# Fetching the row tags by a gather, and waits by block at the edge between two stages

## The chip, the cores and the metric

The kernel runs on one core of one Trainium2 chip. The metric is the device time of one execution in microseconds; the median of three runs stands for a kernel. The profiled execution is one more run, recorded by the hardware profiler. TensorE, VectorE, ScalarE, GpSimd and the queue engine SyncE (SP) each work through their own list of instructions and wait for each other by semaphores.

## The reference

```python
out = attention_scan(q, k, v, a_re, a_im)      # a complex decay scan over 768 steps, 16 heads of 48
x = out.reshape(1536, 384)
# switch layer: 8 experts, each token to its best one, at most 384 tokens per expert
logits = x @ w_gate;  expert = argmax(logits)
gate = softmax(logits)[expert]
h = relu(disp @ w1[e]);  y = h @ w2[e]          # disp: the rows kept by expert e, in order
x = gate * y[expert, pos] if kept else 0        # (1536, 384)
# bilinear layer
return ((x @ w_a) * (x @ w_b)) @ w_out          # 384 -> 1536 -> 384
```

All of it is float32. In the kernel each float32 operand of the large products is split into a high part (h) and the rest (l), and a product is three matmuls (h·h, l·h, h·l).

## The kernel before

Stage 1, up to about 236 us, computes the scan in chunks and the routing of every row. A row goes by an indirect DMA into a DRAM table `sorted_x[expert, rank]` of rows with 386 values: the 384 of x and two **tags**, the sum of the exponentials (its reciprocal is the gate value) and the row's number. Slots that no row takes hold 0 and a number out of range. `total` holds, per expert, how many rows it kept, and `fst`, the place of its first kept row when all kept rows are packed behind each other; `first` and `nkept` are integer copies.

Stage 2 works through the 8 experts. `hidden(e)` is the first product: 8 groups f of 9 matmuls (L1006) with 224 moving columns (384 where an expert has more rows), into four banks in turn; ScalarE writes hh = relu, VectorE hl, and between them they split w2. `outputs(e)` is the second product (L1041): for each f, three column blocks c of three matmuls, into banks 4, 5 and 6, and only after the last of the 72 does `act.wait(m_p)` let ScalarE copy yh and VectorE compute yl, block by block (L1066, L1068), into the packed arrays yh and yl at the column `first[e]`. After f = 1, 3 and 5 TensorE turns one tile of 128 rows of the next expert (`turn_tile`): L943 turns the two tag columns, L945 the three blocks of x. `split_tile` then copies xh (L951), the tags into `tags` at the next expert's place (L952), and xl (L955). Experts 0 to 5 are outputs of a hardware loop (`trip`), 6 follows it with the same body; each prepares the next expert.

SP's queue carries, in the order of the code: the rows of the next expert but one (L907), its w1 (L901) and its w2 (L904), each as soon as the buffer is free. Before the loop it carries w2 of expert 1 and `load_group(0)`, the first of six groups of weights of the bilinear layer.

The last expert's `outputs` turns no tiles. Behind its product TensorE turns `tags` back by 12 small transposes (L1151), and VectorE makes from them `back`, the row numbers, and `gate2`, the squared gate values (L1154 to L1157). All of TensorE's bilinear stage waits for the last yl (`pe.wait(m_y)`), ScalarE's for gate2.

Stage 3, the bilinear layer, takes the packed rows in three tiles of 512. For each of 12 groups f: 18 matmuls (L1208) for a and b, ScalarE copies a (L1221), VectorE multiplies by b (L1223), ScalarE and VectorE split the result (gh L1227, gl L1229), and `outs(f - 1)` adds to the output by 12 matmuls (L1181). In the first tile the weights are split alongside, in the order that they are needed. At the end of a tile ScalarE scales four blocks of 128 rows by gate2 (L1245), and GpSimd scatters each to its rows in DRAM by `back` (L1248).

Key lines around the edge between stages 2 and 3:

```python
            act.wait(m_p)                       # one mark: the whole second product
            for c in range(KC):
                m = act.done(ss.activation(yh[:, c, ...], bank[YB0 + c][:, 0:CAP], ACT.Copy))
...
        m_y = outputs(E - 1, True)
        pe.wait(m_tagged)
        for i in range(NT):
            m = nc.tensor.transpose(tag[:, i, :], tags[:, i * P:(i + 1) * P], ident[0:2, 0:2])
...
            act.wait(m_rows)
            pe.wait(m_y)
```

Of the kernel before, what the change touches and what calls it, by code (L numbers as in the profile page):

```python
# [68 lines left out]
def build(nc, dims, qk, v, a, w_gate, w1, w2, wa, wb, wo, out, CAP):  # L69
# [33 lines left out]
    with ctx:  # L103
# [9 lines left out]
        sorted_x = nc.dram_tensor("sorted_x", (E, N, ROW), F32, kind="Internal").ap()  # L113
        x_rows = nc.dram_tensor("x_rows", (P, L, C2), F32, kind="Internal").ap()
# [51 lines left out]
        with att:  # L166
# [706 lines left out]
            tags = sb("tags", [2, N + CAP], F32, at=exp_r, side="right")  # L873
            used = 2 * KC * (F + CAP) + XT_N * ROW
            assert 2 * KC * F2 <= used and used + N + CAP <= 3 * KC * F2 - GF * KC * P
            sb("apart", [P, 4 * KC * F2 - used - N - CAP], F32, at=exp_r, side="right")
# [51 lines left out]
        extra = sb("raw2", [P, 2 * GA + GO], F32, at=ctx)  # L928
        pool.wait(pe_done, dve_done)
# [33 lines left out]
        act.wait(m_tags)  # L963
# [4 lines left out]
        for i in range(XT_N):  # L968
            m_x0 = split_tile(i, bank[4 + i], m_t0[i], 0)
# [53 lines left out]
        def outputs(e, last):  # L1023
# [8 lines left out]
            m_p = (pe, pe.n + tiles + 1, pe.reg is not None)  # L1032
            m_t = [(pe, pe.n + i + 1, pe.reg is not None) for i in range(tiles)]
            m_x = [(dve, dve.n + 3 * i + 3, dve.reg is not None) for i in range(tiles)]

            def mm(cols):
                for f in range(NF):
                    pe.wait(m_h[f])
                    for c in range(KC):
                        for i, (wx, xx) in enumerate(((w2h, hh), (w2h, hl), (w2l, hh))):  # L1040
                            m = nc.tensor.matmul(bank[YB0 + c][:, 0:cols], wx[:, f, c * P:(c + 1) * P], xx[:, f, 0:cols],  # L1041
                                                 start=f == 0 and i == 0, stop=f == NF - 1 and i == 2)
# [8 lines left out]
            sized(n, mm)  # L1051
# [3 lines left out]
            else:  # L1055
                at_next = nc.scalar.value_load(first[0:1, bass.ds(e + 1, 1)], min_val=0, max_val=N)
                nc.scalar.wait_ge(s_w1, (e + 2) * 16)
                w1_marks[0] = []
                for f in range(NF):
                    w1_marks[0].append(split(*piece1(f)))  # L1060
                    if f % 2 and f // 2 < tiles:
                        assert split_tile(f // 2, bank[7], m_t[f // 2], at_next) == m_x[f // 2]
                row_marks[0] = (m_t[-1], m_x[-1])
            act.wait(m_p)
            for c in range(KC):
                m = act.done(ss.activation(yh[:, c, bass.ds(at_act, CAP)], bank[YB0 + c][:, 0:CAP], ACT.Copy))  # L1066
                dve.wait(m)
                m_y = dve.done(tt(yl[:, c, bass.ds(at_dve, CAP)], bank[YB0 + c][:, 0:CAP],  # L1068
                                  z32(yh[:, c, bass.ds(at_dve, CAP)]), ALU.subtract))
# [29 lines left out]
        load_group(0)  # L1099
        act.wait(m_y0)  # L1100
# [17 lines left out]
        nc_loop(nc, trip, E - 2, (pe, dve, act), {id(pe): NF + 1 + XT_N, id(dve): per, id(act): per + XT_N}, ENG)  # L1118
# [27 lines left out]
        m_tagged = (act, act.n, False)  # L1146
# [158 lines left out]
```

## Time and profile before

| | |
|---|---|
| median of 3 runs | 625.35 us (624.22 to 625.88) |
| profiled execution | 623.43 us, span 622.2 us |
| TensorE busy with matmuls | 560.4 us, 90% of the span |
| VectorE, ScalarE busy | 368.7 us (59%), 274.7 us (44%) |
| GpSimd busy | 40.5 us (7%) |
| mean granted TensorE clock | 0.969 |
| DMA traffic | 70.10 MB, 113 GB/s over the span |

The span runs from the first to the last instruction; the profiled time is the device time of the same execution. Matmuls are pipelined, so the busy time of TensorE is not time at its peak: what a group of them costs is read from start to start.

### The profile page before, as it was taken

The page shows a single profiled execution, that of the slowest core. Times are in us where ns is not written, and L with a number is a line of the kernel's source. Part 1 is how long each engine was busy: PE and PEld are TensorE (multiplying, and loading weights), DVE is VectorE, ACT ScalarE, POOL GpSimd, SP SyncE. Part 2 cuts the span into 40 slices and gives each one's busy share as a digit, 9 for nine tenths or more (in the row PEclk, how much of TensorE's full clock was granted, in tenths as well). Part 3 has the DMA queues.
Part 4 walks back from the last instruction along what each step waited for, and adds up shares of the span by engine and source line. Part 5 has one row for each costly group of instructions (what it writes and reads, how often), then busy time and mean ns, then how long its engine had stood idle before and what let it go on. Part 6 is the DMA issues. An engine that isn't in the chain of part 4 may idle for free.

```text
span 622.2 us, 10348 instructions
## 1 busy us (share of the span) xinstructions
PE 560.4 (90%) x3876; PEld 496.6 (80%) x3877; DVE 368.7 (59%) x910; ACT 274.7 (44%) x571; POOL 40.5 (7%) x51
## 2 busy tenths in 40 slices
PE   0564878899999986999999999999999999999996
PEld 0232555899999984999999998888888888888886
DVE  5999999777667645888888876444422222121211
ACT  5656475712222224777877775443332121321112
POOL 1000000001111116000000000000001000110002
PEclk9867899999999988999999999899999999999999
DMA  8990035493222115566677734222001000010001
GB/s 334 397 337 1 2 152 146 133 309 83 65 62 58 41 30 171 167 241 194 217 239 240 222 123 154 76 77 76 1 1 51 1 0 1 14 39 1 0 1 51
DMA packets 42201, 70.10 MB, mean 113 GB/s; under 512 B 12976, under 2 KB 35248, under 8 KB 41456
## 3 DMA queue, kind: packets, MB, share of 16 engines
q1 hardware_dynamic: 40624, 64.80, 31.7%
q0 software_dynamic: 1536, 4.73, 2.4%
q8 instruction: 28, 0.46, 0.3%
q14 instruction: 13, 0.11, 0.1%
HBM read 52.97 MB, written 16.55 MB: 112 GB/s over the span
## 4 chain that ended last, share of the span: by engine, by line
PE 80%; DVE 13%; ACT 3%; DMA 2%; issue 1%; POOL 0%; SPq 0%; DVEq 0%; ACTq 0%; POOLq 0%
PE psum L1208 25%; PE psum L1181 12%; PE psum L1006 10%; PE psum L1041 10%; PE psum L815 4%; PE psum L649 4%; PE psum L789 3%; DVE region L357 3%; PE psum L819 2%; PE psum L442 2%; DVE region L362 2%; PE psum L834 2%; PE psum L690 1%; DVE region L406 1%; PE psum L945 1%
## 5 line engine op out<-in xcount | busy, mean ns | idle before, releaser
L1223 DVE TENSOR_TENSOR ga<-ga,psum 128x512 f32<-128x512 f32 x36 | 24.8, 688 | 134.1 <-PE psum L1208 134.1
L1227 ACT ACTIVATE gh<-ga 128x512 fp32r<-128x512 f32 x36 | 22.8, 632 | 82.4 <-DVE ga L1223 77.9
L265 PE MATMUL psum<-region,ident 128*128 128x384 f32 (+1 forms) x42 | 23.3, 646 | 39.4 <-ACT region L275 28.4
L1221 ACT ACTIVATE ga<-psum 128x512 f32<-128x512 f32 x36 | 21.5, 598 | 76.3 <-PE psum L1208 76.3
L1041 PE MATMUL psum<-hh,w2h 128*128 128x224 f32 x192 | 54.1, 282 | 0.0
L1006 PE MATMUL psum<-xh,w1h 128*128 128x224 f32 x192 | 52.9, 275 | 1.3 <-DVE xl L955 1.3
L1006 PE MATMUL psum<-xh,w1l 128*128 128x224 f32 x192 | 52.8, 275 | 0.8 <-issue 0.8
L1006 PE MATMUL psum<-xl,w1h 128*128 128x224 f32 x192 | 52.7, 274 | 0.0
L1041 PE MATMUL psum<-hh,w2l 128*128 128x224 f32 x192 | 52.6, 274 | 0.0
L1041 PE MATMUL psum<-hl,w2h 128*128 128x224 f32 x192 | 52.5, 273 | 0.0
L265 PEld LDWEIGHTS psum<-region,ident 128*128 128x128 f32 x42 | 10.3, 262 | 48.6 <-issue 21.0
L1181 PE MATMUL psum<-woh,gh 128*128 128x384 f32 x144 | 48.6, 338 | 0.4 <-DVE gl L1229 0.2
L1181 PE MATMUL psum<-wol,gh 128*128 128x384 f32 x144 | 48.6, 337 | 0.0
L1181 PE MATMUL psum<-woh,gl 128*128 128x384 f32 x144 | 48.3, 336 | 0.0
L1208 PE MATMUL psum<-yh,wah 128*128 128x512 f32 x108 | 43.2, 400 | 1.5 <-DVE yl L1068 1.5
L1208 PE MATMUL psum<-yh,wal 128*128 128x512 f32 x108 | 43.2, 400 | 0.0
L1208 PE MATMUL psum<-yl,wah 128*128 128x512 f32 x108 | 43.1, 399 | 0.0
L1208 PE MATMUL psum<-yh,wbh 128*128 128x512 f32 x108 | 42.9, 398 | 0.0
L1208 PE MATMUL psum<-yl,wbh 128*128 128x512 f32 x108 | 42.8, 397 | 0.0
L1208 PE MATMUL psum<-yh,wbl 128*128 128x512 f32 x108 | 42.7, 395 | 0.0
L1229 DVE TENSOR_TENSOR gl<-ga,gh 128x512 fp32r<-128x512 f32 x36 | 25.0, 693 | 25.2 <-ACT gh L1227 25.2
L1006 PEld LDWEIGHTS psum<-xh,w1h 128*128 128x128 f32 x192 | 36.9, 192 | 1.6 <-DVE xl L955 1.6
(185 smaller groups left out, 1475.3 us busy)
## 6 DMA issues: line engine op xcount, KB each, us to landing
raw<-w SPq DMA_DIRECT2D x14, 1536.0 KB, 6.9
sorted_x<-region SPq DMA_DIRECT2D x8, 579.0 KB, 11.2
queries<-qk SPq DMA_DIRECT2D x4, 1152.0 KB, 17.4
xrow<-sorted_x SPq DMA_DIRECT2D x7, 579.0 KB, 3.9
region<-x_rows SPq DMA_DIRECT2D x14, 288.0 KB
queries<-w SPq DMA_DIRECT2D x2, 1536.0 KB, 10.8
x_rows<-region SPq DMA_DIRECT2D x5, 576.0 KB, 2.8
region<-a SPq DMA_DIRECT2D x2, 1152.0 KB, 8.6
```

What stands on the lines that cost most here:

```text
L265: nc.tensor.matmul(x, ident[:], x0[:, cut], start=True, stop=False)
L357: m.append(dve.done(tt(by[k_], walk(AT_Z[2] + prev + k_ * D, [-SA, 2], [0, 2], [1, D]), walk(AT_Z[0] + now + k_ * D, [SA, 2], [SA, 2], [1, ...
L649: m = nc.tensor.matmul(bank[2 + r][0:L, i * L:(i + 1) * L], XT[:, p, :], QT[:, p, :], start=True, stop=True)
L815: m = nc.tensor.matmul(bank[4 + r][0:L, i * D:(i + 2) * D], SC[r][:, i, :], twice(p), start=True, stop=j == 0)
L1006: m = nc.tensor.matmul(bank[b][:, 0:cols], wx[:, c, f * P:(f + 1) * P], xx[:, c, 0:cols], start=c == 0 and i == 0, stop=c == KC - 1 and i ...
L1041: m = nc.tensor.matmul(bank[YB0 + c][:, 0:cols], wx[:, f, c * P:(c + 1) * P], xx[:, f, 0:cols], start=f == 0 and i == 0, stop=f == NF - 1 ...
L1181: m = nc.tensor.matmul(ot[s][:, 0:DM], gx[f % GB3][:, s * P:(s + 1) * P], wx[:, f, :], start=f == 0 and i == 0, stop=f == NF2 - 1 and i == 2)
L1208: m = nc.tensor.matmul(b_[:, 0:TT], wx[:, f, c, :], xx[:, c, t * TT:(t + 1) * TT], start=c == 0 and i == 0, stop=c == KC - 1 and i == 2)
L1221: m = act.done(ss.activation(ga[f % 2][:], ba[:, 0:TT], ACT.Copy))
L1223: m = dve.done(tt(ga[f % 2][:], ga[f % 2][:], bb[:, 0:TT], ALU.mult))
L1227: m = act.done(ss.activation(gh[f % GB3][:], ga[f % 2][:], ACT.Copy))
L1229: m_g.append(dve.done(tt(gl[f % GB3][:], ga[f % 2][:], z32(gh[f % GB3][:]), ALU.subtract)))
```

## The change

The tags are no longer carried through TensorE. After expert 0's first product SP's queue copies them out of `sorted_x` into a small DRAM table `kept_tags` of 8 x 384 pairs. During the last expert's copies VectorE works out for each packed row its place in that table: the row's own packed number plus, for each expert whose rows end before it, the slots which that expert left free (`skip`). GpSimd then gathers the pairs by 12 indirect DMAs, and VectorE makes `back` and `gate2` from them in step 10 of the first bilinear tile. The second product of the last expert goes through its second half block by block, with a mark for each; the copies yh and yl wait by block, and so does the first bilinear product.

```diff
+        kept_tags = nc.dram_tensor("kept_tags", (E, CAP, 2), F32, kind="Internal").ap()
...
-            tags = sb("tags", [2, N + CAP], F32, at=exp_r, side="right")
...
-        m_tags = pool.done(g.memset(tags[:], FAR))
         g.wait_ge(s_sc, 16 * TAU)
+        pool.done(g.memset(tag[:], FAR))
+        m_at = pool.done(g.iota(at_row[:], pattern=[[P, NT]], base=0, channel_multiplier=1,
+                                allow_small_or_imprecise_dtypes=True))
...
         def turn_tile(i, b):
-            nc.tensor.transpose(b[0:2, KC * P:(KC + 1) * P], xrow[:, i, DM:ROW], ident[:])
...
-        def split_tile(i, b, m_turned, at):
+        def split_tile(i, b, m_turned):
             act.wait(m_turned)
-            act.done(ss.activation(xh[:, :, i * P:(i + 1) * P], s_, ACT.Copy))
-            m = act.done(ss.activation(tags[:, i * P:N + (i + 1) * P][:, bass.ds(at, P)], b[0:2, KC * P:(KC + 1) * P],
-                                       ACT.Copy))
+            m = act.done(ss.activation(xh[:, :, i * P:(i + 1) * P], s_, ACT.Copy))
...
-            m_p = (pe, pe.n + tiles + 1, pe.reg is not None)
+            m_p = [(pe, pe.n + (c + 1 if last else tiles + 1), pe.reg is not None) for c in range(KC)]
...
+            def by_block(cols):
+                for f in range(NF // 2):
+                    pe.wait(m_h[f])
+                    for c in range(KC):
+                        w2_mm(cols, f, c)
+                for c in range(KC):
+                    for f in range(NF // 2, NF):
+                        pe.wait(m_h[f])
+                        m = w2_mm(cols, f, c)
+                    assert pe.done(m) == m_p[c]
...
-            sized(n, mm)
+            sized(n, by_block if last else mm)
...
-                at_next = nc.scalar.value_load(first[0:1, bass.ds(e + 1, 1)], min_val=0, max_val=N)
...
-            act.wait(m_p)
+            m_y = []
             for c in range(KC):
+                act.wait(m_p[c])
...
         load2(1)
         load_group(0)
+        s_kept = sem("s_kept")
+        sp.dma_start(kept_tags, sorted_x[:, 0:CAP, DM:ROW]).then_inc(s_kept, 16)
...
-        pe.wait(m_tagged)
-        tag = bank[7][:, 0:2 * NT].rearrange("p (i c) -> p i c", c=2)
+        kept, fst = total[:, :, 0], total[:, :, 2]
+        dve.wait(m_at)
+        dve.done(vv.tensor_copy(edge[:, 0:E - 1], fst[:, 1:E]))
+        dve.done(tt(edge[:, E - 1:E], fst[:, E - 1:E], kept[:, E - 1:E], ALU.add))
+        dve.done(vv.tensor_scalar(skip[:, 0:E - 1], kept[:, 0:E - 1], -1.0, float(CAP), ALU.mult, ALU.add))
+        m = dve.done(vv.memset(skip[:, E - 1:E], float(2 * E * CAP)))
+        dve.wait(m)
+        D_(tt(past[:], at_row[:].unsqueeze(2).broadcast_to([P, NT, E]),
+              edge[:].unsqueeze(1).broadcast_to([P, NT, E]), ALU.is_ge))
+        D_(tt(past[:], past[:], skip[:].unsqueeze(1).broadcast_to([P, NT, E]), ALU.mult))
+        D_(vv.tensor_reduce(out=gate2[:], in_=past[:], axis=AXX, op=ALU.add))
+        D_(tt(gate2[:], gate2[:], at_row[:], ALU.add))
+        m = dve.done(vv.tensor_copy(source[:], gate2[:]))
+        s_tag = sem("s_tag")
+        pool.wait(m)
+        g.wait_ge(s_kept, 16)
         for i in range(NT):
-            m = nc.tensor.transpose(tag[:, i, :], tags[:, i * P:(i + 1) * P], ident[0:2, 0:2])
+            g.indirect_dma_start(out=tag[:, i, :], out_offset=None, in_=kept_tags.rearrange("e n k -> (e n) k"),
+                                 in_offset=bass.IndirectOffsetOnAxis(ap=source[:, i:i + 1], axis=0),
+                                 bounds_check=E * CAP - 1, oob_is_err=False).then_inc(s_tag, 16)
...
-            act.wait(m_rows)
-            pe.wait(m_y)
...
                         for c in range(KC):
+                            if first_tile and f == 0:
+                                pe.wait(m_y[c])
...
+                    if first_tile and f == NF2 - 2:
+                        vv.wait_ge(s_tag, 16 * NT)
+                        dve.done(vv.tensor_copy(back[:], tag[:, :, 1]))
+                        D_(vv.tensor_scalar(gate2[:], tag[:, :, 0], 1e-9, None, ALU.add))
+                        D_(vv.reciprocal(gate2[:], gate2[:]))
+                        m_rows = D_(tt(gate2[:], gate2[:], gate2[:], ALU.mult))
```

The memory layout changes with it: `tags` goes, some small arrays of at most 96 columns come.

## Rows read from the trace of the kernel before

**Rows 1.** Page part 4 (engine shares), then the chain: start us, us, engine, line.

```profile
PE 80%; DVE 13%; ACT 3%; DMA 2%; issue 1%; POOL 0%; SPq 0%; DVEq 0%; ACTq 0%; POOLq 0%
...
268.03 0.85 issue
...
360.20 2.01 PE psum L1041 x18
362.65 2.00 PE psum L1041 x18
...
387.92 10.21 PE psum L1208 x36
398.13 2.10 PE psum L1181 x12
...
465.77 8.40 PE psum L1208 x36
```

**Rows 2.** Timeline, all engines, edge between stages 2 and 3: start, duration, instruction.

```profile
385.34 0.27 PE L1041 MATMUL psum<-hh,w2l 128*128 128x224 f32 x1
...
385.74 1.26 ACT L1066 ACTIVATE yh<-psum 128x384 f32 x3 [5.57 <-PE psum L1041]
386.37 1.49 DVE L1068 TENSOR_TENSOR yl<-psum,yh 128x384 f32 x3 [4.97 <-ACT yh L1066]
```

**Rows 3.** Stretches: length, engines' busy time, granted clock, DMA share, GB/s.

```profile
385.50:387.90 2.40, 0.95 (x13) 0.82 (x12) 1.53 (x5) 1.26 (x3) 0.00 (x0) 1.00 0.98 334
...
389.00:390.00 1.00, 1.00 (x4) 0.81 (x3) 0.80 (x2) 0.93 (x3) 0.00 (x0) 0.50 0.00 0
...
393.00:394.00 1.00, 1.00 (x6) 0.77 (x6) 0.00 (x0) 0.00 (x0) 0.00 (x0) 1.00 0.00 0
```

**Rows 4.** Timeline of TensorE, then of VectorE, in the last trip.

```profile
362.05 0.27 PE L943 MATMUL psum<-ident,xrow 128*2 128x128 f32 x1
362.16 0.49 PE L945 MATMUL psum<-ident,xrow 128*128 128x128 f32 x3
...
376.18 0.55 DVE L890 TENSOR_TENSOR w2l<-raw,w2h 128x384 fp32r<-128x384 f32 x1
376.65 0.55 DVE L1017 SCALAR_TENSOR_TENSOR hl<-psum,hh 128x384 fp32r<-128x384 f32 x1
```

**Rows 5.** Timeline, all engines, last row tile of expert 0.

```profile
245.21 0.49 ACT L951 ACTIVATE xh<-psum 128x384 fp32r<-128x384 f32 x1 [0.89 <-PE psum L945]
245.60 0.25 ACT L952 ACTIVATE tags<-psum 2x128 f32<-2x128 f32 x1
245.88 0.56 DVE L955 TENSOR_TENSOR xl<-psum,xh 128x384 fp32r<-128x384 f32 x1 [0.97 <-ACT tags L952]
```

**Rows 6.** Group of a small VectorE operation (busy us, mean ns); timeline of GpSimd.

```profile
L362 DVE TENSOR_TENSOR region<-region 128x96 f32<-128x96 f32 x94 | 19.8, 252 | 0.0
```

```profile
466.95 0.99 POOL L1248 DMA_INDIRECT out<-raw,back  x1 [0.30 <-issue]
```

**Rows 7.** Stretches of trip 0 and timeline of trip 1, all engines.

```profile
269.00:271.00 2.00, 2.00 (x18) 1.98 (x19) 1.30 (x4) 1.52 (x4) 0.00 (x0) 1.00 0.90 365
271.00:273.00 2.00, 2.00 (x21) 2.00 (x20) 2.00 (x5) 1.80 (x5) 0.00 (x0) 1.00 0.08 25
...
275.08 0.94 ACT L888 ACTIVATE w1h<-raw 128x384 fp32r<-128x384 f32 x2 [0.79 <-issue]
...
276.58 0.55 DVE L955 TENSOR_TENSOR xl<-psum,xh 128x384 fp32r<-128x384 f32 x1
...
277.64 0.27 PE L943 MATMUL psum<-ident,xrow 128*2 128x128 f32 x1
```

**Rows 8.** Stretches around w_gate's load; DMA queue 1, 159 to 166: packets, MB, share.

```profile
25.00:25.60 0.60, 0.00 (x0) 0.00 (x0) 0.60 (x4) 0.57 (x2) 0.00 (x0) 1.00 0.95 399
25.60:26.40 0.80, 0.00 (x0) 0.00 (x0) 0.34 (x3) 0.80 (x2) 0.00 (x0) 1.00 0.99 278
...
q1 hardware_dynamic: 784, 0.29, 18.0%
```

More of the change, by code:

```diff
@@ L872, in build @@
             xrow = sb("xrow", [P, XT_N, ROW], F32, at=exp_r, side="right")
-            tags = sb("tags", [2, N + CAP], F32, at=exp_r, side="right")
             used = 2 * KC * (F + CAP) + XT_N * ROW
-            assert 2 * KC * F2 <= used and used + N + CAP <= 3 * KC * F2 - GF * KC * P
-            sb("apart", [P, 4 * KC * F2 - used - N - CAP], F32, at=exp_r, side="right")
+            assert 2 * KC * F2 <= used <= 3 * KC * F2 - GF * KC * P
+            sb("apart", [P, 4 * KC * F2 - used], F32, at=exp_r, side="right")
             w2h, w2l = (sb(n_, [P, NF, DM], F32R, at=exp_r, side="right") for n_ in ("w2h", "w2l"))
@@ L928, in build @@
         extra = sb("raw2", [P, 2 * GA + GO], F32, at=ctx)
+        at_row = sb("at_row", [P, NT])
+        past = sb("past", [P, NT, E])
+        source = sb("source", [P, NT], I32)
+        tag = sb("tag", [P, NT, 2])
+        skip, edge = (sb(n_, [P, E]) for n_ in ("skip", "edge"))
         pool.wait(pe_done, dve_done)
-        m_tags = pool.done(g.memset(tags[:], FAR))
         g.wait_ge(s_sc, 16 * TAU)
+        pool.done(g.memset(tag[:], FAR))
+        m_at = pool.done(g.iota(at_row[:], pattern=[[P, NT]], base=0, channel_multiplier=1,
+                                allow_small_or_imprecise_dtypes=True))
         for x in (yh, yl):
@@ L962, in build @@
         pe.wait(m_first)
-        act.wait(m_tags)
         m_t0 = []
@@ L1031, in outputs, with w2_mm @@
             tiles = 0 if last else XT_N
-            m_p = (pe, pe.n + tiles + 1, pe.reg is not None)
+            m_p = [(pe, pe.n + (c + 1 if last else tiles + 1), pe.reg is not None) for c in range(KC)]
             m_t = [(pe, pe.n + i + 1, pe.reg is not None) for i in range(tiles)]
             m_x = [(dve, dve.n + 3 * i + 3, dve.reg is not None) for i in range(tiles)]
+            def w2_mm(cols, f, c):
+                for i, (wx, xx) in enumerate(((w2h, hh), (w2h, hl), (w2l, hh))):
+                    m = nc.tensor.matmul(bank[YB0 + c][:, 0:cols], wx[:, f, c * P:(c + 1) * P], xx[:, f, 0:cols],
+                                         start=f == 0 and i == 0, stop=f == NF - 1 and i == 2)
+                return m
+            def by_block(cols):
[8 more added lines that the diff above has]
+                    assert pe.done(m) == m_p[c]
             def mm(cols):
@@ L1039, in mm @@
                     for c in range(KC):
-                        for i, (wx, xx) in enumerate(((w2h, hh), (w2h, hl), (w2l, hh))):
-                            m = nc.tensor.matmul(bank[YB0 + c][:, 0:cols], wx[:, f, c * P:(c + 1) * P], xx[:, f, 0:cols],
-                                                 start=f == 0 and i == 0, stop=f == NF - 1 and i == 2)
+                        m = w2_mm(cols, f, c)
                     i = f // 2
@@ L1117, in build @@
         per = 2 * NF + NF + KC + XT_N
-        nc_loop(nc, trip, E - 2, (pe, dve, act), {id(pe): NF + 1 + XT_N, id(dve): per, id(act): per + XT_N}, ENG)
+        nc_loop(nc, trip, E - 2, (pe, dve, act), {id(pe): NF + 1 + XT_N, id(dve): per, id(act): per}, ENG)
         def split_ab(f):
@@ L1145, in build @@
             lazy[n_] = sb(n_, [P, NF2, KC, P], F32R, at=bl, side="right")
-        m_tagged = (act, act.n, False)
         m_y = outputs(E - 1, True)
-        pe.wait(m_tagged)
-        tag = bank[7][:, 0:2 * NT].rearrange("p (i c) -> p i c", c=2)
-        for i in range(NT):
-            m = nc.tensor.transpose(tag[:, i, :], tags[:, i * P:(i + 1) * P], ident[0:2, 0:2])
-        m = pe.done(m)
-        dve.wait(m)
-        dve.done(vv.tensor_copy(back[:], tag[:, :, 1]))
-        D_(vv.tensor_scalar(gate2[:], tag[:, :, 0], 1e-9, None, ALU.add))
-        D_(vv.reciprocal(gate2[:], gate2[:]))
-        m_rows = D_(tt(gate2[:], gate2[:], gate2[:], ALU.mult))
+        kept, fst = total[:, :, 0], total[:, :, 2]
[14 more added lines that the diff above has]
+        g.wait_ge(s_kept, 16)
+        for i in range(NT):
+            g.indirect_dma_start(out=tag[:, i, :], out_offset=None, in_=kept_tags.rearrange("e n k -> (e n) k"),
+                                 in_offset=bass.IndirectOffsetOnAxis(ap=source[:, i:i + 1], axis=0),
+                                 bounds_check=E * CAP - 1, oob_is_err=False).then_inc(s_tag, 16)
         exp_l.close()
@@ L1189, in outs @@
                         pe.wait(m_start)
-                        if first_tile:
-                            pe.wait(m_rows)
                     if first_tile:
@@ L1244, in tile @@
                     act.wait(m_end[s])
+                    if first_tile:
+                        act.wait(m_rows)
                     m = act.done(ss.activation(os_[s], ot[s][:, 0:DM], ACT.Copy,
                                                scale=gate2[:, t * NS + s:t * NS + s + 1]))
-                    pool.wait(m, m_rows)
+                    pool.wait(m)
                     g.indirect_dma_start(out=out[:, :],
```

8 lines of the change are left out of this document (4 added, 4 removed).

## The prediction

> **What bounds the kernel now.** I read three views in this order: the chain of work that ended last, the timeline around the two places that the diff touches, and the stretches by granted clock and DMA share. The chain is TensorE for 80% of the span [rows 1], so what counts is TensorE time and the gaps between its matmuls. In the expert loop the chain never leaves TensorE: the second product goes in pieces of 18 matmuls, 2.00 us each, that start 2.44 us apart [rows 1], and what fills the other 0.44 us is one tile of row transposes. Every wait that ScalarE and VectorE show in the loop is therefore theirs alone. TensorE stops only at the edges of the stage: before the first product of expert 0, and between the last product of expert 7 and the bilinear stage.
>
> The second edge is dear. The last expert matmul starts at 385.34, the three blocks of its result are then copied (yh on ScalarE from 385.74) and subtracted (yl on VectorE, 386.37 to 387.86), and the first bilinear matmul starts at 387.92 [rows 2]. After that gap the granted clock, 1.00 within it, stands at 0.50 (1.2 GHz) from 389 to 390 and is back at 1.00 (2.4 GHz) from 393 to 394 [rows 3]. The price shows in the chain: the first 36 bilinear matmuls take 10.21 us, the same 36 at the start of the next tile 8.40 us [rows 1]. So gap and slow clock together cost about 4.3 us.
>
> **The change, part by part.** (1) *No tag transposes in the loop.* Each of the three row tiles of a trip loses one L943 transpose. It starts at 362.05 and its successor at 362.16 [rows 4]: 0.11 us. TensorE works without a gap there, so it is on the path. Seven calls (experts 0 to 6 prepare experts 1 to 7) with three tiles are 21 x 0.11 = 2.3 us. ScalarE loses three tag copies and one register load per trip, VectorE's xl no longer waits for the tag copy; neither was last, so I cost them at nothing. A trip gets 0.33 us shorter, and ScalarE and VectorE have to keep up: VectorE's busiest part is 16 operations of 0.47 us pitch [rows 4], 7.5 us, in a first product of 8.04 us, which still fits.
>
> (2) *Expert 0.* There the last row tile is on the path: L943 is 0.11 us as in the loop; then xh runs 245.21 to 245.70, the tag copy from 245.60 to 245.85, and xl starts at 245.88 [rows 5]. Without the copy xl can start 0.03 us behind xh, at 245.73: 0.15 us. Together 0.26 us.
>
> (3) *Block order in the last second product.* The first half (f = 0 to 3) stays as it is. The second half goes block by block: 12 matmuls at 2.00/18 = 0.111 us, 1.34 us for each c. Blocks 0 and 1 are finished 2.68 and 1.34 us ahead of block 2. All inputs are ready, since the last split of w2 is long done then. The copy of block c starts 0.40 us behind the start of its last matmul and the subtraction 0.63 us behind that [rows 2], so yl of block 0 is there at about 384.2, of block 1 at 385.6, of block 2 at 386.92. The bilinear product now waits by block: it starts at 385.45, behind the last expert matmul, and comes to its block 2 after six matmuls of 8.40/36 = 0.233 us, at 386.85, where it stands still for some 0.1 us. With a start-up of 0.05 us the gain against 387.92 is 2.3 us. The 12 tag transposes (L1151) that lay in the gap are gone, hidden before and hidden now.
>
> (4) *Clock.* With the gap goes what lowered the clock: TensorE does full-size matmuls without a pause over a tenth of a microsecond. I count the whole 10.21 - 8.40 = 1.8 us.
>
> (5) *Index arithmetic on VectorE.* Nine small operations behind yl. A 128x96 one takes 252 ns [rows 6]; two of that size, one reduction, and six shorter ones come to about 2 us, 386.9 to 389. Queued behind them are wol, wal, wbl (1.4 us, to 390.4) and then ga of the first step, which could start at about 389.9. So ga starts some 0.5 us late. It is hidden: its user is the first output product, which in the chain starts one whole ab product (4.2 us) behind the first ab [rows 1], here about 394, and ga, gh and gl need 2.1 us. If that cover were gone it would cost 0.5 us. On ScalarE woh no longer waits for the gate values, which brings it forward.
>
> (6) *The gather.* Twelve indirect DMAs on GpSimd, priced by the twelve of the output: 0.99 us each and 0.30 between [rows 6], 15.5 us from 389 to 405. GpSimd has nothing else until the first output, some 60 us later; VectorE waits for the tags only in step 10 of 12 (about 450). The four small gate operations there (under 1 us) lie in VectorE's idle time. Cost nothing.
>
> (7) *The copy of the tags to the small table.* This is the one term that the trace can't price well. It is a DRAM to DRAM copy of 8 x 384 pairs, 8 bytes each, so 3072 tiny pieces, on SP's queue behind w2 of expert 1 and weight group 0, and ahead of the rows and of w1 of expert 2. The DMA engines are full there until 271.0 (share 0.90, then 0.08) [rows 7]. What stands behind it in the queue lands later by as much as it takes. ScalarE begins to split w1 of expert 2 at 275.08, VectorE's xl of row tile 0 ends at 277.13, and TensorE's second tile of transposes, which waits for it, comes at 277.64 [rows 7]. TensorE will be some 0.7 us earlier there, the chain from load to xl 0.15 us shorter: w1 may land up to 275.0, so 4.0 us of delay are free, and each one beyond stops TensorE. The price of a tiny piece: nearest in size are the 384 pieces of 32 bytes of w_gate. Over 0.8 us the traffic falls from 399 to 278 GB/s [rows 8]; less their own 12 KB that is 0.27 us of all 16 engines, 11.4 ns a piece. Upper bound: 784 packets, nearly all of 384 bytes, take 18.0% of 16 engines in 7 us [rows 8], 25.7 ns each. The copy is then 35 to 79 us of one engine: spread over all sixteen 2.2 to 4.9 us, over half of them 4.4 to 9.9 us. A piece of 8 bytes is nearer to 32 than to 384, so I take 11.4 ns; the delay of 2.2 to 4.4 us is then all but hidden, a stall of 0 to 0.4 us. I put in 0.2. No row shows a small write into DRAM, so the price can be higher.
>
> The Trainium skill, "DMA: Bandwidth & Descriptors", section "Queues, rings and completion order" and what follows it on the semaphore increment, says that a DMA is split over the largest number of engines up to 16 that divides the slowest dimension of both sides; that dimension is 8 here, so half of the engines would carry it all. By that rule the delay is 4.4 us (stall 0.4) at the low price and 9.9 us at the high one. No row of this trace shows a copy with such a shape.
>
> **Sum.** -2.3 (loop) -0.26 (expert 0) -2.3 (gap) -1.8 (clock) +0.2 (copy) = -6.5 us. The profiled execution took 623.43 us (span 622.2), 1.9 under the median of the three runs, 625.35; the sum is from its own rows, and I apply it to the median: 618.9 us. What a measurement can tell here is 0.3%, 1.9 us.
>
> **Rivals.**
> *A, as summed (chance 0.50):* 618.9, own range 617.4 to 620.0.
> *B, the copy costs part of the gain (0.18):* pieces of 14 to 22 ns on eight engines delay by 5.4 to 8.4 us, a stall of 1.4 to 4.4 us, and a stop over 2 us may bring a slow clock as at the other edge: 620 to 624, middle 622.
> *C, slower, one mechanism (0.16):* the load of w1 of expert 2 is held up in the queue. At 25.7 ns on eight engines the stall is 5.9 us plus 1.8 us of slow clock, 7.7 us: 625.35 - 6.7 + 7.7 = 626.4. The point from which it takes all is a delay of 8.9 us, which is 23 ns a piece on eight engines or 46 ns on sixteen; a loss that can be measured begins at 28 ns on eight. For it: the DMA engines are full until 271, and nothing in this trace writes 8 bytes into DRAM. Against it: the 32-byte row.
> *D, the clock falls all the same (0.09):* some remaining stop near 386 is enough. Then 1.8 us are not gained: 620.7.
> *E, TensorE waits for its code (0.07):* the chain has 0.85 us of "issue" at 268.03, in full DMA traffic [rows 1]; the bilinear code is reached while weight groups are loading too. A stop there was covered by the gap and would now show: 619.8.
> That the change doesn't do what it says would need a wait on block 2 in front of the bilinear product; the first triple uses block 0 alone, so I give it nothing of its own.
>
> **Numbers.** Faster by over 0.3% (under 623.5): A, D, E and most of B, 0.78. Within 0.3%: the rest of B and the mild end of C, 0.11. Slower (over 627.2 or close to it by C's heavier prices): 0.11. Range: below A's 617.4 I allow for a run like the fastest (624.22 - 6.7 = 617.5) and a little more, 617.2; above it reaches through B into C, 625.0, which leaves out less than 2 in 10.
>
> **What would show it.** Loop: in the chain the pieces of 18 start 2.33 us apart, TensorE without gaps. Edge: first L1208-like matmul within 0.2 us of the last second product, the first 36 in 8.4 to 8.5 us, granted clock 1.00 at 389. Copy: SP's DMA at about 259; ScalarE's first w1 split in trip 1 near 274.5 without "DMA" as its releaser, and TensorE's second tile of transposes unhindered. If ScalarE there waits for raw, or xl comes late and TensorE stands at about 277, B or C holds. The prediction is wrong most easily in (7), next in (4).

## The result, and the profile after

| | before | after |
|---|---|---|
| median | 625.35 us (621.00 to 625.88, 5 runs) | 635.14 us (632.26 to 636.86, 5 runs) |
| ratio, 95% interval | | 1.0166 (1.0121 to 1.0211) |
| profiled execution | 623.43 us, span 622.2 | 632.26 us, span 631.0 |
| mean granted clock | 0.969 | 0.961 |

The change makes the kernel slower by 9.8 us. 618.9 us with a range up to 625.0 was predicted: the sign is wrong.

The chain of work of after, from the first expert of the loop to the third. The line L951 is the transposes of the rows, L1009 the first product, L1041 the second:

```profile
265.89 4.04 PE psum L1009 x36
...
273.02 17.21 DMA raw<-w
...
292.37 0.55 PE psum L951 x3
292.91 2.01 PE psum L1041 x18
...
295.25 2.00 PE psum L1041 x18
297.25 8.04 PE psum L1009 x72
305.29 2.01 PE psum L1041 x18
...
307.63 2.01 PE psum L1041 x18
```

In the kernel before the chain never left TensorE in the loop [rows 1]. Here it leaves it once: the load of w1 of expert 2, issued at 273.02, lands 17.2 us later. The waits from 262 to 300 us (total, times, longest) say what each engine stood for:

```profile
ACT w1h L888 <- DMA raw<-w: 15.4, 1, 15.4
...
PE psum L951 <- DMA xrow<-sorted_x: 10.5, 1, 10.5
```

SP's timeline shows the copy of the tags in front of these two loads, and what it does to the issue of the next:

```profile
261.16 0.90 SPq L1119 DMA_DIRECT2D kept_tags<-sorted_x  x1
264.15 8.53 SPq L907 DMA_DIRECT2D xrow<-sorted_x  x1
273.02 3.10 SPq L901 DMA_DIRECT2D raw<-w  x1
```

And the stretches, where the last two columns are the DMA share and GB/s, the one before them the granted clock:

```profile
268.00:270.00 2.00, 2.00 (x21) 2.00 (x20) 2.00 (x6) 1.80 (x6) 0.00 (x0) 1.00 1.08 3
...
274.00:276.00 2.00, 1.94 (x18) 1.76 (x16) 1.61 (x4) 0.88 (x2) 0.00 (x0) 1.00 0.53 4
276.00:278.00 2.00, 0.00 (x0) 0.00 (x0) 0.00 (x0) 0.00 (x0) 0.00 (x0) 1.00 0.87 26
278.00:280.00 2.00, 0.00 (x0) 0.00 (x0) 0.00 (x0) 0.00 (x0) 0.00 (x0) 1.00 0.99 39
280.00:282.00 2.00, 0.00 (x0) 0.00 (x0) 0.00 (x0) 0.00 (x0) 0.00 (x0) 0.75 1.03 48
282.00:284.00 2.00, 0.00 (x0) 0.00 (x0) 0.00 (x0) 0.00 (x0) 0.00 (x0) 0.50 0.61 61
284.00:286.00 2.00, 0.00 (x0) 0.00 (x0) 0.00 (x0) 0.00 (x0) 0.00 (x0) 0.50 0.89 290
```

The reader is to see two things. From 268 to 276 the DMA engines are busy and move next to nothing: these are the 8-byte pieces, the last of which start at 277.1. And from 278 to 284, when the pieces are gone and the rows go through (1544 bytes each), they still move only 39 to 61 GB/s, where the DMA engines reach 365 in the kernel before [rows 7]. ScalarE begins with w1 of expert 2 at 290.26 and not at 275.08 [rows 7], 15.2 us later, and TensorE stands from 276 to 286, first for the rows, and then runs at 0.50 of its clock; the wait that ends last is that for w1, so it sets the loss.

The other edge went as meant. The chain from the last second product on:

```profile
390.55 8.04 PE psum L1041 x72
398.58 8.64 PE psum L1235 x36
407.23 2.11 PE psum L1208 x12
```

From the start of the last second product to the first output product it is 16.68 us, where it was 20.56 us before (from 377.57 to the 398.13 of [rows 1]). The gather, meant to be hidden, is:

```profile
L1184 POOL DMA_INDIRECT tag<-kept_tags,source x12: 996/1032/1187, 402.3 to 417.4; - x12
```

One thing was not foreseen. The first product of expert 0 took 9.82 us in the chain of after, where before it took 8.30:

```profile
247.06 9.82 PE psum L1009 x72
```

The granted clock (the last column but two) shows why: it stands at 0.50 here, and at 1.00 in the same stretches of the kernel before.

```profile
247.00:248.00 1.00, 0.94 (x4) 0.94 (x5) 0.01 (x1) 0.00 (x0) 1.00 (x1) 0.50 1.00 414
...
249.00:250.00 1.00, 1.00 (x7) 1.00 (x7) 0.12 (x1) 0.64 (x2) 0.43 (x1) 0.50 1.08 390
```

The difference of the spans, 8.8 us, by sections of the chain: up to the first product of expert 0 +0.6; from there to the last second product +12.4 (the stop +14.0, that slow product +1.5, the rest are the shorter trips and a wait of 0.85 us that is gone); the edge -3.9; what follows -0.3.

### The profile page after: what moved, and what is told of

Its sections match the earlier page's. It is cut to its first block, busy times and chain, and to the rows that moved or that the text cites. A ratio compares the mean times of both kernels' runs of the same rounds, so it can differ in the third digit from the quotient of the medians.

```text
span 631.0 us, 10240 instructions
## 1 busy us (share of the span) xinstructions
PE 560.2 (89%) x3840; PEld 495.4 (79%) x3841; DVE 369.9 (59%) x919; ACT 272.0 (43%) x547; POOL 51.8 (8%) x64
## 4 chain that ended last, share of the span: by engine, by line
PE 77%; DVE 14%; DMA 4%; ACT 3%; issue 1%; POOL 0%; SPq 0%; DVEq 0%; POOLq 0%; ACTq 0%
PE psum L1235 24%; PE psum L1208 11%; PE psum L1009 10%; PE psum L1041 10%; PE psum L816 4%; PE psum L650 4%; DVE region L358 3%; PE psum L790 3%; DMA raw<-w 3%; PE psum L820 2%; DVE region L363 2%; PE psum L443 2%; PE psum L835 2%; PE psum L691 1%; DVE region L407 1%
## 5 line engine op out<-in xcount | busy, mean ns | idle before, releaser
L1041 PE MATMUL psum<-hh,w2h 128*128 128x224 f32 x192 | 55.1, 287 | 0.0
L1009 PE MATMUL psum<-xh,w1h 128*128 128x224 f32 x192 | 53.5, 279 | 1.2 <-DVE xl L959 1.2
L1041 PE MATMUL psum<-hl,w2h 128*128 128x224 f32 x192 | 53.5, 279 | 0.0
L1041 PE MATMUL psum<-hh,w2l 128*128 128x224 f32 x192 | 53.5, 279 | 0.0
L1009 PE MATMUL psum<-xl,w1h 128*128 128x224 f32 x192 | 53.4, 278 | 0.0
L1009 PE MATMUL psum<-xh,w1l 128*128 128x224 f32 x192 | 53.3, 278 | 0.0
L1256 DVE TENSOR_TENSOR gl<-ga,gh 128x512 fp32r<-128x512 f32 x36 | 24.9, 693 | 25.2 <-ACT gh L1254 25.2
L890 DVE TENSOR_TENSOR w1l<-raw,w1h 128x384 fp32r<-128x384 f32 x56 | 28.6, 552 | 17.8 <-ACT w1h L888 17.7
## 6 DMA issues: line engine op xcount, KB each, us to landing
sorted_x<-region SPq DMA_DIRECT2D x8, 579.0 KB, 11.2
queries<-w SPq DMA_DIRECT2D x2, 1536.0 KB, 12.4
```

The lines of the kernel that those rows point to most:

```text
L890: return dve.done(tt(dst_l, src, z32(dst_h), ALU.subtract))
L1009: m = nc.tensor.matmul(bank[b][:, 0:cols], wx[:, c, f * P:(f + 1) * P], xx[:, c, 0:cols], start=c == 0 and i == 0, stop=c == KC - 1 and i ...
L1256: m_g.append(dve.done(tt(gl[f % GB3][:], ga[f % 2][:], z32(gh[f % GB3][:]), ALU.subtract)))
```

## The experiments

All medians of before on the chips of the experiments are 623.4 to 623.9 us.

**e1: the copy alone, in the kernel before.** Its result is not used by anything.

```diff
+        kept_tags = nc.dram_tensor("kept_tags", (E, CAP, 2), F32, kind="Internal").ap()
...
         load_group(0)
+        s_kept = sem("s_kept")
+        sp.dma_start(kept_tags, sorted_x[:, 0:CAP, DM:ROW]).then_inc(s_kept, 16)
...
+            sp.wait_ge(s_kept, 16)
```

> The kernel before with nothing but the copy of the tags added, at the changed kernel's place; nothing reads its result. Theory 1 (the copy holds up the rows and w1 of expert 2, and nothing else of the change costs anything): the second product of expert 1 takes 14 us longer, as in the changed kernel, where it went from 9.3 to 23.3 us, so the time is 625.4 + 14 = about 639 us, with the same long DMA issue on SP's queue and a stop of TensorE before the row transposes. Rival 2 (the stop needs the rest of the change too, for instance the shorter trip or a shifted DMA order): a stop of 5 us or less, 625 to 631 us.

Measured: 639.40 us, ratio 1.025 (1.0217 to 1.0283). The waits repeat those of after:

```profile
ACT w1h L889 <- DMA raw<-w: 14.8, 1, 14.8
...
PE psum L944 <- DMA xrow<-sorted_x: 9.9, 1, 9.9
```

The copy alone costs 15.6 us of the median, as theory 1 has it. The loss is the copy, and the rest of the change must bring 5 to 6 us.

**e2: the changed kernel with the copy behind the loop** and behind weight groups 1 and 2.

```diff
         load_group(0)
-        s_kept = sem("s_kept")
-        sp.dma_start(kept_tags, sorted_x[:, 0:CAP, DM:ROW]).then_inc(s_kept, 16)
...
         for i in range(1, NRING):
             load_group(i)
+        s_kept = sem("s_kept")
+        sp.dma_start(kept_tags, sorted_x[:, 0:CAP, DM:ROW]).then_inc(s_kept, 16)
```

> The changed kernel with the copy moved behind the loop and behind the weight groups 1 and 2, where no load of an expert stands behind it. Theory 1: the stop in trip 1 is gone, TensorE works through the loop in trips of 17.05 us, the edge keeps its gain: 625.4 - 6.5 = 619 us, or 620.5 if the slow clock at 247 that the changed kernel shows stays. The copy then lands at about 405 us and the gathers behind it at about 420; weight group 3 comes behind the copy in the queue and is needed at about 411, which is where it could cost 1 to 3 us. Rival 2 (the gather or the index arithmetic costs something of its own): 622 us or more with a stop in the bilinear stage.

Measured: 619.58 us, ratio 0.9937 (0.9911 to 0.9963). No stop in the loop, the edge at 16.70 us as in after, and the first product of expert 0 again slow. The copy is as slow here as it was there (its pieces start from 385.8 to 396.8), as the stretches show:

```profile
388.00:390.00 2.00, 2.00 (x10) 1.59 (x10) 1.20 (x3) 0.48 (x1) 0.00 (x0) 1.00 0.76 3
...
394.00:396.00 2.00, 2.00 (x12) 1.77 (x10) 1.60 (x4) 1.61 (x4) 0.00 (x0) 1.00 0.32 4
396.00:398.00 2.00, 2.00 (x10) 1.63 (x9) 0.49 (x2) 0.60 (x1) 0.00 (x0) 1.00 0.99 33
...
402.00:404.00 2.00, 2.00 (x10) 1.58 (x10) 0.79 (x2) 0.58 (x1) 0.42 (x1) 1.00 0.57 95
```

But TensorE is busy for 2.00 of 2.00 us in each of them: weight group 3, which crawls behind the copy, has time. So it is the place that costs, given the price.

**What makes the copy slow: e3 to e6, e10, e11.** Each changes one property of it, e6 two. e5 differs from e1 also in the number of DMAs, so it is to be compared with e3.

e3 makes eight copies of 384 pairs, one per expert, so that the slowest dimension is 384 and not 8:

```diff
-        sp.dma_start(kept_tags, sorted_x[:, 0:CAP, DM:ROW]).then_inc(s_kept, 16)
+        for e in range(E):
+            sp.dma_start(kept_tags[e], sorted_x[e, 0:CAP, DM:ROW]).then_inc(s_kept, 16)
...
-        g.wait_ge(s_kept, 16)
+        g.wait_ge(s_kept, 16 * E)
```

> The changed kernel with the copy cut into eight, one for each expert, so that the outermost dimension of each is 384 instead of 8; the same 3072 pieces of 8 bytes. Theory A (half of the DMA engines carry all pieces, each at about 43 ns): spread over all engines the copy takes half as long, 8 instead of 16 us, the stop of TensorE shrinks from 14 to about 5 us: 626 us. Theory B (the pieces are limited where they are written, not by the engine that carries them): the copy takes as long as before, 634 us.

e4 keeps the one copy and puts the pairs of the table 64 bytes apart (and fills the table with zeros in stage 1):

```diff
-        kept_tags = nc.dram_tensor("kept_tags", (E, CAP, 2), F32, kind="Internal").ap()
+        kept_tags = nc.dram_tensor("kept_tags", (E, CAP, 16), F32, kind="Internal").ap()
...
-        sp.dma_start(kept_tags, sorted_x[:, 0:CAP, DM:ROW]).then_inc(s_kept, 16)
+        sp.dma_start(kept_tags[:, :, 0:2], sorted_x[:, 0:CAP, DM:ROW]).then_inc(s_kept, 16)
```

> The changed kernel with a table whose pairs lie 64 bytes apart instead of 8, filled with zeros in stage 1 by one more contiguous store of 196 KB; the copy has the same 3072 pieces. Theory C (neighbouring pieces fall into one line of the memory and wait for each other there): the pieces are quick, the stop goes, about 620 us. Theory A or D (each piece costs the same wherever it lands): no change, 633 to 636 us.

e5 is e1 with the same 3072 pieces of 8 bytes, read from the same places, but into SBUF:

```diff
+        in_sbuf = sb("in_sbuf", [P, E * XT_N, 2], at=ctx)
...
+        s_kept = sem("s_kept")
+        for e in range(E):
+            sp.dma_start(in_sbuf[:, e * XT_N:(e + 1) * XT_N, :],
+                         sorted_x[e, 0:CAP, DM:ROW].rearrange("(i p) k -> p i k", p=P)).then_inc(s_kept, 16)
```

> The kernel before plus an unused copy of the same 3072 tag pairs, read in the same 8-byte pieces from the same rows and at the same place of SP's queue, but written into SBUF (eight DMAs of 384 pairs) instead of DRAM; nothing else differs. Theory W (small writes into DRAM are what is dear): the load behind it lands almost in time, TensorE doesn't stop in trip 1, 624 to 626 us, as before. Rival R (each 8-byte piece costs the same wherever it goes, since it is the read or the descriptor that is dear): the rows come as late as with eight copies into DRAM, TensorE stops for 6 us or more, 631 to 640 us.

e6 has both the eight copies of e3 and the 64 bytes of e4:

> The changed kernel with both remedies together: eight copies of 384 pairs, one per expert, and a table whose pairs stand 64 bytes apart. Each alone shortened the stop at the rows from 10.5 us to 6.4 and 2.4 us. Theory M (the two act on different things, number of engines and writes that meet in one line, and multiply): the copy takes 5 to 6 us, TensorE does not stop in trip 1 or for under 1 us, 620 to 622 us. Rival N (both act on the same limit, so the second adds nothing): stop of 2 us or more, 626 to 628 us.

e10 is after with the same copy on GpSimd's queue, at the same time:

```diff
-        sp.dma_start(kept_tags, sorted_x[:, 0:CAP, DM:ROW]).then_inc(s_kept, 16)
+        pool.wait(m_w2)
+        g.dma_start(kept_tags, sorted_x[:, 0:CAP, DM:ROW]).then_inc(s_kept, 16)
```

> The changed kernel with the same single copy at the same time, but issued by GpSimd on its own queue, behind a wait for the same split that SP's load of weight group 0 waits for. Theory O (what costs is that the rows stand behind the copy in one queue's order): the rows land as early as before, TensorE does not stop at 276, 619 to 621 us. Rival T (the small pieces hold the DMA engines or the memory themselves, whichever queue they come from): the rows still come 5 us late or more, 626 to 635 us.

e11 is e1 with the pairs of four experts, half of the pieces:

```diff
+        s_kept = sem("s_kept")
+        sp.dma_start(kept_tags[0:4], sorted_x[0:4, 0:CAP, DM:ROW]).then_inc(s_kept, 16)
```

> The kernel before plus an unused copy as in e1, but of experts 0 to 3 alone: 4 x 384 pairs, half of the pieces. The Trainium skill, page DMA: Bandwidth & Descriptors, section Queues, rings and completion order, would put them on four engines by the slowest dimension of 4. Theory S (each engine works off its own 384 pieces and that sets the time): copy as long as in e1, rows 10 us late, 637 to 640 us. Rival M (the number of pieces in all sets it, in the memory or in the queue): half the delay, TensorE's stop under 5 us, 626 to 632 us.

Measured; the two waits are the longest of TensorE for the rows and of ScalarE for w1, in us, as the waits of each trace have them:

| | base | median us | ratio (95%) | wait for rows | wait for w1 |
|---|---|---|---|---|---|
| e1 one copy | before | 639.40 | 1.025 (1.0217 to 1.0283) | 9.9 | 14.8 |
| e11 half the pieces | before | 636.09 | 1.0188 (1.0135 to 1.024) | 7.9 | 12.9 |
| e5 into SBUF | before | 628.60 | 1.0081 (1.0054 to 1.0108) | none | 4.8 |
| e10 GpSimd's queue | after | 639.26 | 1.0255 (1.0205 to 1.0305) | 11.0 | 15.9 |
| e3 eight copies | after | 630.58 | 1.0121 (1.0065 to 1.0177) | 6.4 | 11.2 |
| e4 64 bytes apart | after | 627.51 | 1.0044 (1.002 to 1.0069) | 2.4 | 7.5 |
| e6 both | after | 627.70 | 1.0075 (1.0045 to 1.0104) | 1.6 | 6.5 |

In e5 and e6 TensorE then stands another 3.4 us for xl, behind w1. The times of e3 fall into two pairs, 627.9 and 633.3 to 633.7 us; its trace, and so its two waits, belong to the faster pair.

What single packets did, from the same traces: the 8-byte pieces, and the 384 packets of the rows that come next (in the kernel before these took 67 ns in the mean, 180 at most). The median of the 8-byte pieces is 9 ns in every line.

| | pieces start, us | mean and longest, ns | rows: mean and longest, ns |
|---|---|---|---|
| after | 267.3 to 277.1 | 44, 3056 | 321, 2659 |
| e1 one copy | 267.2 to 276.9 | 44, 2659 | 298, 2714 |
| e11 half the pieces | 268.1 to 277.7 | 38, 3561 | 215, 3627 |
| e4 64 bytes apart | 269.5 to 274.3 | 18, 1294 | 172, 2455 |
| e3 eight copies | 265.6 to 272.2 | 9, 224 | 216, 2525 |
| e6 both | 268.0 to 273.1 | 9, 127 | 127, 1939 |
| e5 into SBUF | 266.8 to 271.1 | 9, 28 | 85, 811 |

So the small piece is not dear as such, into DRAM no more than into SBUF. In after 157 of the 3072 take over 200 ns, and these stalls make the copy long.

e11: the DMA counts of two stretches of 10 us, the first of e1 from 267 to 277 us, the second of e11 from 268 to 278:

```profile
DMA packets 3248, 0.29 MB, mean 29 GB/s; under 512 B 3096, under 2 KB 3246, under 8 KB 3246
...
q1 hardware_dynamic: 3246, 0.26, 101.2%
```

```profile
DMA packets 1717, 0.29 MB, mean 29 GB/s; under 512 B 1556, under 2 KB 1715, under 8 KB 1715
...
q1 hardware_dynamic: 1715, 0.26, 62.2%
```

Half of the pieces fill the same time, with 62% of the engines' time instead of 101%. That fits a count for each engine: 384 in both, 25 to 26 ns a piece (10 us over 384), which is a mean over quick pieces and stalls and not what a piece takes. The rule of the Trainium skill, "DMA: Bandwidth & Descriptors", section "Why a DMA increments its semaphore by 16 and not by 1", gives eight and four engines for slowest dimensions of 8 and 4; the trace names no engines, only the length agrees. These two runs alone don't show that the time grows with the pieces of one engine. e11's median of 636.09 lies in neither theory's range, nearer to the 637 to 640 of S than to the 626 to 632 of M, and its waits are 2 us shorter than those of e1.

e3: with eight copies of 384 the pieces lie within 6.6 us (265.6 to 272.2) and don't stall; they come about as fast as SP issues the eight DMAs (8.96 us). Whether it is a spread over more engines or the cut into eight that ends the stalls is open, and a single DMA of all the pieces into SBUF was not run. Its median of 630.58 us lies between theory A (626) and B (634). But then the rows crawl, while in e5, where the same reads go to SBUF, they don't. First two stretches of e3, then two of e5:

```profile
272.00:274.00 2.00, 2.00 (x20) 2.00 (x20) 1.99 (x5) 1.16 (x3) 0.00 (x0) 1.00 0.92 51
274.00:276.00 2.00, 0.33 (x3) 0.14 (x2) 0.00 (x0) 0.00 (x0) 0.00 (x0) 1.00 0.68 42
```

```profile
270.00:272.00 2.00, 1.84 (x15) 1.83 (x16) 1.74 (x4) 1.24 (x3) 0.00 (x0) 1.00 0.46 36
272.00:274.00 2.00, 2.00 (x20) 2.00 (x19) 1.92 (x5) 1.80 (x5) 0.00 (x0) 1.00 1.00 349
```

So the slow traffic behind the copy goes with the small writes into DRAM. With 64 bytes between the pairs (e4, 627.51 us, between theory C's 620 and the 633 to 636 of A and D) both stalls and slow rows are less; e4 still has both. The rival in e5 is not empty, though: 628.6 us is far from the 624 to 626 of theory W. Its timeline of SP shows what is left:

```profile
260.36 9.39 SPq L1103 DMA_DIRECT2D in_sbuf<-sorted_x  x8
270.30 0.39 SPq L907 DMA_DIRECT2D xrow<-sorted_x  x1
```

SP needs 9.39 us to issue eight DMAs of 384 pieces, 1.17 us each, and the rows are issued 12.2 us behind the load of w2 (258.06 to 270.30), in the kernel before 6.0 us behind it (256.40 to 262.38). e6 has the same price (9.20 us for its eight), so it could hardly get below it: the number of rival N of e6 came true, but in the main by a third limit that neither theory had named. Its rows also still took 6.9 us to land, against 3.9 in e5.

e10: the queue's order is not it. SP issues the rows at 264.93 there and is not held, and yet they land 25.2 us later, at 290.1 (in after at 286.4):

```profile
PE psum L951 <- DMA xrow<-sorted_x: 14.1, 3, 11.0
```

Theory O is refuted; rival T's mechanism held, above its range of 626 to 635 us. GpSimd's queue sends the copy in another form, as 96 packets of 256 and 512 bytes from 265.6 to 282.3, and the first packet of the rows starts at 282.6. So the copy holds the DMA engines or the memory for whoever comes next, also from the other queue. The Trainium skill, "DMA: Bandwidth & Descriptors", section "Back-pressure in remote DMA", says of another kind of transfer (remote DMA) that stalled writes also stall the other queues of the engine that makes them. e10 looks like that; whether it is the same mechanism no run shows.

**e7: a bridge over TensorE's pause at expert 0.** e2, with three matmuls more in front of the first product (their result is not used).

```diff
+        for i in (0, 1, 2):
+            nc.tensor.matmul(bank[i][:, 0:CAP], ident[:], ident[:].unsqueeze(1).broadcast_to([P, XT_N, P]),
+                             start=True, stop=True)
```

> The changed kernel with the copy moved behind the loop, plus three matmuls of 128x384 (their result unused) between the row transposes of expert 0 and its first product, so that TensorE pauses less there. Theory P (the slow clock at 247 to 250, which made that product 9.9 us instead of 8.3, follows from the pause before it): granted clock 1.00 through 247 to 250, first product of expert 0 at about 8.3 us, 617.5 to 618.5 us, ratio to the kernel before 0.989 to 0.991. Rival Q (the clock falls there for another reason, or the matmuls themselves lie on the path and cost what they bring): product still near 9.9 us or the gain eaten, 619 to 620.5 us.

Measured: 616.85 us, ratio 0.9901 (0.9879 to 0.9924), the best of all. The chain:

```profile
243.79 0.55 PE psum L951 x3
244.34 1.94 PE psum L972 x6
246.27 8.03 PE psum L1012 x72
```

From the end of the row transposes to the end of that product it takes 9.97 us (244.34 to 254.31), in e2 11.09 (245.46 to 256.55). The granted clock is 1.00 throughout, as theory P has it; the median lies below its 617.5 to 618.5, the ratio within its 0.989 to 0.991. The median is 2.7 us lower than that of e2 (2.2 by the ratios, each to the kernel before on its own chip), of which these 1.1 us are explained. Over all traces the picture is this: in the profiled executions of after, e2, e4, e8, e9 and e10, which turn no tags, the product took 9.8 to 11.3 us, and e3 and e6, where it is broken by a wait, ran at 0.21 to 0.23 us a matmul too (8.30 over 72 is 0.115); of the four kernels with tag transposes, before, e1 and e5 had 8.30 and e11 10.64; both kernels with the bridge had 8.03. So work in the pause kept the clock in both traces that have the bridge. Without it the tag transposes go along with the full clock in three traces of four and their absence with the slow one in eight of eight; that they are the cause is not shown.

**e8, e9, e12: what the two waits by block are worth.** e8 is e2 with the old order in the last second product; e9 also lets the bilinear stage wait for all three blocks; e12 is e9 with the bridge of e7. The last pair of lines is in e9 and e12 only.

```diff
-            m_p = [(pe, pe.n + (c + 1 if last else tiles + 1), pe.reg is not None) for c in range(KC)]
+            m_p = [(pe, pe.n + tiles + 1, pe.reg is not None) for c in range(KC)]
...
-            sized(n, by_block if last else mm)
+            sized(n, mm)
...
-                                pe.wait(m_y[c])
+                                pe.wait(*m_y)
```

> The changed kernel with the copy behind the loop, but the last expert's second product in the old order (not by block), the waits of the bilinear stage by block kept. Theory G (the gap and the slow clock behind it both come back): the first bilinear matmul starts some 2 us after the last expert matmul, granted clock 0.50 for a few us, the first 36 bilinear matmuls 10.2 us instead of 8.7, 623 to 624 us. Rival H (without the tag transposes and with waits by block the gap is shorter and the clock stays): the block order brings 1.5 us or less, 620 to 621.5 us.

> The kernel of e8 (old order of the last second product, copy behind the loop), and the bilinear stage now waits for all three blocks of yh and yl before its first matmul, as the kernel before does; only the 12 tag transposes in the gap are missing against before. In e8 the gap was 1.45 us and the granted clock stayed at 1.00. Theory L (the length of the gap lowers the clock): gap 2.3 to 2.7 us, clock 0.50 behind it, the first 36 bilinear matmuls about 10.2 us, 623 to 624 us. Rival K (the gap alone does not lower it; what stood in the gap before, the 2-column transposes, or chance did): gap 2.3 to 2.7 us, the first 36 matmuls still 8.7 us, 621.5 to 622.5 us.

> The kernel of e7 (copy behind the loop, three matmuls in the pause of expert 0), with the edge of e9: old order of the last second product and one wait for all three blocks. Against e7, which had a median of 616.85 us, it prices the two waits by block together, without the slow clock at 247 in either. e9 showed a gap of 2.4 us behind which the granted clock stayed at 1.00. Theory K (a gap of that length alone does not lower the clock): first 36 bilinear matmuls again 8.6 to 8.7 us, 619.0 to 619.6 us. Rival L (e9 was chance, the clock usually falls behind such a gap, as it did in the kernel before): the first 36 take 10.2 us, 620.5 to 621.5 us.

Measured: e8 621.15 us, ratio 0.9962 (0.9941 to 0.9982); e9 623.26, 0.9992 (0.9967 to 1.0017); e12 622.40, 0.9971 (0.9942 to 1.0), both without one run of 949.42 us at a mean granted clock of 0.571. e8 is as rival H has it. e9's median lies in theory L's range, but its trace is K's: the clock stayed at 1.00 behind the gap. e12 lies above both of its ranges. The chains of e8, e9 and e12, from the last second product to the first output product:

```profile
376.22 8.05 PE psum L1041 x72
...
385.72 8.64 PE psum L1235 x36
394.37 2.09 PE psum L1208 x12
```

```profile
379.57 8.05 PE psum L1041 x72
...
390.01 8.62 PE psum L1235 x36
398.63 2.08 PE psum L1208 x12
```

```profile
376.73 8.05 PE psum L1044 x72
...
387.17 10.18 PE psum L1238 x36
397.35 2.11 PE psum L1211 x12
```

The section takes 16.70 us in e2, 18.15 in e8, 19.06 in e9 and 20.62 in e12, and in e12 all of the last step is the clock. (The kernel before, with its 12 tag transposes in the gap, had 20.56, so these cost nothing.) So of the 3.9 us at this edge the order by block brings 1.45, the wait by block 0.9, and the clock 1.55, where it is lost. Between e12 and e7, which differ by the two waits, the ratios differ by 0.0070, 4.4 us. The clock is not always lost: behind a gap of 2.3 to 2.4 us the first 36 matmuls took 10.2 us in before, e1, e11 and e12 and 8.6 us in e5 and e9. With a gap of 1.45 us (e8) or none they took 8.64 to 8.66 in every trace that shows one. e9 taken alone spoke for theory K, e12 against it; together they say that the gap makes the slow clock possible, and what decides between the two is open.

## Why the prediction was wrong

**The step that failed is (7)**, the copy of the tags, entered at +0.2 us. What it said about the slack of w1 was right: w1 could land up to 275.0, 4.0 us late, and each microsecond beyond stopped TensorE (w1 landed 15.2 us past that limit, 0.6 of it since all of after starts that much later here, and TensorE lost 14.0 us). It set no such limit for the rows, which stand in front of w1 in the queue; they landed at 286.4 instead of 269.0 and stopped TensorE first, for 10.5 us, but w1's wait ended last. The delay was mis-sized: w1 landed at about 290.3, some 19 us later than the 271.0 of before, and TensorE's stop came to 14.0 us. In the step's own unit, a price per piece on eight engines, I took 11.4 ns with 25.7 ns as the upper bound; 19.3 us over 384 are 50 ns.

Two things were wrong in it, and both are stalls and not a price per piece. I argued that 8 bytes are nearer to 32 than to 384, and took the price of the row of w_gate, a load into SBUF. For the single piece that was right: its median is 9 ns. But the one copy into DRAM stalls, and comes to 25 to 26 ns a piece on eight engines in the mean; that this meets my upper bound is luck, since that bound came from larger pieces that did not stall so. The other half had no place in the bounds at all: the loads behind the copy went at 39 to 61 GB/s for 6 us, and SP was held for 8.53 us at the issue of the rows, so that it issued w1 at 273.02 instead of 264.55. I had written that no row shows a small write into DRAM and that the price could be higher, and still let the range end where the rows for loads ended. With 25.7 ns alone rival C gives 626.4; the measured 635.1 lies outside of all that I had worked out. Rival C is what happened, in mechanism and place, at twice its price, with a chance of 0.16. That was low for a price that no row showed.

**(1) The loop**: right. The pieces start 2.34 us apart (305.29, 307.63), predicted 2.33. From the first product of expert 0 to the last second product e7 takes 128.29 us (246.27 to 374.56), in before it is 131.08 us (246.49 to 377.57): -2.8 us, against -2.3 predicted. The rest is not from the transposes: the first product took 8.03 us instead of 8.30, and the "issue" of 0.85 us at 268.03 [rows 1] is 0.64 us in e7.

**(2) Expert 0**: from the landing of the rows to the first matmul it is 1.76 us (245.30 to 247.06), in before 1.96 (244.53 to 246.49): -0.20 us of the -0.26. But the step overlooked the clock behind them. The product went from 8.30 to 9.82 us. The transposes in the pause of TensorE had been costed as work that is in the way; e7 shows that work there can pay, since the clock stayed at 1.00 behind it.

**(3) and (4) The edge**: right in sum, -3.9 against -4.1. The split was -2.3 and -1.8; e8, e9 and e12 give about -2.35 and -1.55, the latter where the clock had fallen at all, and less because the first 36 matmuls take 8.64 us at full clock and not the 8.40 of the next tile. I took the fall as certain; in two of six traces it doesn't come behind the gap.

**(5) and (6)**: right. The index arithmetic and the twelve gathers (1032 ns each, 402.3 to 417.4) are hidden; what follows the edge takes 0.3 us less than before.

Without its step (7) the prediction was -6.7 us. e2 has -4.3 us of medians (-5.5 of spans) and e7 -6.6 (-7.2 of spans): the gain that was worked out is there, once the copy is out of the way of the rows and the lost clock at expert 0 is bridged.

## What to carry to other kernels

Before a small DMA is put in front of loads with a few microseconds of slack, count its pieces and ask whether they are written into DRAM; if no row of the trace shows such a write, the range has to be open at the top, and the cheapest remedy is another place in the queue, where nothing soon needed stands behind it. GpSimd's queue instead of SP's didn't help, and cutting it into eight DMAs moved a good part of the price to their issue. And where TensorE pauses before a long product, look at the granted clock there before and after the change: a few matmuls in the pause may be worth more than they cost. A gather straight from `sorted_x`, which would need no copy, was not tried.

## What was not expected of the hardware

- One DMA of 3072 pieces of 8 bytes from DRAM to DRAM took about 10 us on the engines, and the traffic behind it stayed at 39 to 61 GB/s for 6 us more (after). The median piece took 9 ns; 157 of them took over 200 ns, up to 3.1 us. The same pieces into SBUF, as eight DMAs, were followed at once by 349 GB/s (e5).
- Pairs 64 bytes apart in the target shortened TensorE's wait for the rows from 10.5 to 2.4 us (e4). Why the distance matters is open: partial writes that meet in one line of the memory are a guess that no run isolates.
- SP needs 1.12 to 1.17 us to issue a DMA of 384 pieces (8.96, 9.20 and 9.39 us for eight), and one issued behind a large one can take 8.53 us.
- Behind the same gap of 2.3 to 2.4 us TensorE's clock fell to 0.50 in four traces and stayed at 1.00 in two.
